# Keys kept on chip, scores read from them in two pieces, loads reordered, and one batch's value sums moved

## The reference

```
k_sum = k.reshape(B,H,nb,32,D).max(axis=3);  v_sum = v.reshape(B,H,nb,32,D).mean(axis=3)
scores_l = scale * q @ k.T      kept where |i-j| < 16, else -1e9
scores_s = scale * q . k_sum + log(32)
a = softmax(concat(scores_l, scores_s));  x = a @ concat(v, v_sum)
x = (silu(x @ w_gate) * (x @ w_val)) @ w_out          # 512 -> 1536 -> 512
h = x @ w_in;  out = g(h) @ w_out2                    # 512 -> 2048 -> 512
```

## Time and profile before

| | us |
|---|---|
| median of 3 runs | 648.65 |
| span of the profiled execution (the page names no other time of it) | 649.1 |
| PE busy | 627.6 |
| DVE, ACT, POOL busy | 356.3, 323.3, 30.4 |
| PE busy from 90 us to the last matmul | without a gap |

### The profile page before, as it was taken

One profiled execution on the slowest core, in us unless ns is written; L12 is line 12 of the kernel. 1 busy time (PEld: TensorE's weight loads), 2 busy tenths in 40 slices (PEclk: granted clock), 3 DMA queues, 4 the chain that ended last, 5 costly groups with the idle time before them and its releaser, 6 DMA issues.

```text
span 649.1 us, 9400 instructions
## 1 busy us (share of the span) xinstructions
PE 627.6 (97%) x3144; PEld 510.9 (79%) x3144; DVE 356.3 (55%) x553; ACT 323.3 (50%) x622; POOL 30.4 (5%) x33
## 2 busy tenths in 40 slices
PE   5779989999999999999999999999999999999997
PEld 2648868888888888888888888888888888888885
DVE  6855455544455555445333447666666666666664
ACT  1844576773468686434333344444444444444442
POOL 3310000100010101000000000000000000000000
PEclk9989979999999999999999999999999999999999
DMA  9997936512922221322332223232253332333221
GB/s 282 261 308 215 223 98 149 160 54 99 253 97 70 75 88 57 97 98 97 97 97 97 65 66 97 97 97 97 97 164 97 97 97 97 125 134 97 97 81 65
DMA packets 49780, 78.51 MB, mean 121 GB/s; under 512 B 16481, under 2 KB 21601, under 8 KB 49505
## 3 DMA queue, kind: packets, MB, share of 16 engines
q1 hardware_dynamic: 49760, 78.27, 39.8%
HBM read 72.48 MB, written 3.15 MB: 117 GB/s over the span
## 4 chain that ended last, share of the span: by engine, by line
PE 88%; SPq 5%; DMA 3%; DVE 1%; ACT 1%; issue 1%; DVEq 0%; ACTq 0%
PE bank L409 49%; PE bank L472 20%; PE bank L454 14%; DMA v_tok<-v_rows_dram 2%; PE bank L344 2%; PE bank L335 2%; SPq L207 2%; DMA win_raw<-w_dram 1%; SPq L203 1%; PE bank L328 1%; PE bank L321 1%; SPq L226 1%; DVE k_sum L681 1%; SPq L233 0%; ACT prob L536 0%
## 5 line engine op out<-in xcount | busy, mean ns | idle before, releaser
L409 PE MATMUL bank<-x_hi,win_hi 128*128 128x512 f32 (+1 forms) x480 | 191.6, 399 | 0.0
L409 PE MATMUL bank<-x_lo,win_hi 128*128 128x512 f32 (+1 forms) x480 | 188.1, 392 | 0.0
L409 PE MATMUL bank<-x_hi,win_lo 128*128 128x512 f32 (+1 forms) x480 | 187.8, 391 | 0.0
L593 ACT ACTIVATE hid_hi<-v_tok 128x512 fp32r<-128x512 f32 x84 | 53.0, 631 | 128.4 <-DVE v_tok L804 75.5
L409 PEld LDWEIGHTS bank<-x_lo,win_hi 128*128 128x128 f32 x480 | 90.7, 189 | 19.4
L409 PEld LDWEIGHTS bank<-x_hi,win_hi 128*128 128x128 f32 x480 | 90.7, 189 | 19.2 <-issue 0.2
L409 PEld LDWEIGHTS bank<-x_hi,win_lo 128*128 128x128 f32 x480 | 90.7, 189 | 18.3 <-issue 0.2
L774 DVE TENSOR_TENSOR hid_lo<-v_tok,hid_hi 128x512 fp32r<-128x512 f32 x84 | 65.5, 780 | 56.1 <-ACT hid_hi L593 56.0
L764 DVE TENSOR_TENSOR win_lo<-win_raw,win_hi 128x512 fp32r<-128x512 f32 (+1 forms) x84 | 76.9, 916 | 19.5 <-ACT win_hi L569 19.5
L472 PE MATMUL bank<-wout_hi,hid_hi 128*128 128x512 f32 x192 | 74.8, 389 | 0.3 <-ACT hid_hi L593 0.3
L472 PE MATMUL bank<-wout_hi,hid_lo 128*128 128x512 f32 x192 | 74.8, 390 | 0.0
(11 more groups left out here) (54 smaller groups left out, 576.4 us busy)
## 6 DMA issues: line engine op xcount, KB each, us to landing
wout_raw<-w_dram SPq DMA_DIRECT2D x84, 256.0 KB, 2.6
win_raw<-w_dram SPq DMA_DIRECT2D x36, 512.0 KB, 4.1
win_raw<-w_dram SPq DMA_DIRECT2D x48, 256.0 KB, 3.0
k_slot<-k_t_dram SPq DMA_DIRECT2D x24, 192.0 KB, 4.7
v_slot<-v_rows_dram SPq DMA_DIRECT2D x24, 192.0 KB, 5.2
v_tok<-v_rows_dram SPq DMA_DIRECT2D x4, 768.0 KB, 8.9
out_dram<-v_slot SPq DMA_DIRECT2D x12, 256.0 KB, 3.0
k_raw<-k_t_dram SPq DMA_DIRECT2D x2, 1056.0 KB, 12.1
```

The costliest lines, as they stand in the source:

```text
L409: last = nc.tensor.matmul(dst[:], a, m, start=k == 0 and i == 0, stop=k == KD - 1 and i == 2)
L593: nc.scalar.activation(hid_hi[:, r], hid[:, r], ACT.Copy).then_inc(hid_hi_ready, 1)
```

## The change

- The keys of both batches get tiles of their own (`k_all`), loaded in three pieces a batch; `k_raw`, `k_slot`, the 24 key DMAs, `place_k_sum` and `load_k_sum` go.
- `scores` makes two products for each pair: 96 columns from `k_all`, 32 from `k_sum`, with the same queries as weights.
- The block maxima are three reductions a batch.
- Load order: keys, first queries, values. The first batch's value sums follow the scores of tiles 1, 2 and 3, and ACT copies them behind the exponentials of tile 3. SP's two `load_v_sum` stay in its list.
- The second batch's values go to `v_late`; their sums come behind the two products of chunk 0.
- Clearing `q_slot` moves from DVE to POOL; the mask has 3 patterns in place of 12; the engines' `Fori` loops are written out.

```diff
-            def load_v_tok(b):
-                if b:
-                    sp.wait_ge(v_sum_done, b)
+            def load_k(b, c):
+                lo, hi = KCH[c]
+                src = k_t[b, :, lo * PAIRS * SUB:hi * PAIRS * SUB]
+                sp.dma_start(k_all[:, b, lo:hi].rearrange("p c a j -> p (c a j)"), src).then_inc(k_loaded[b][c], 16)
...
-            load_v_tok(0)
-            load_k_raw(0, 0)
-            load_k_raw(0, 1)
-            load_qk(0, 0, 2, qk_first_loaded[0])
-            load_qk(0, 2, GRP)
-            load_qk(1, 0, 2, qk_first_loaded[1])
+            load_k(0, 0)
+            load_k(0, 1)
+            load_k(0, 2)
+            load_q(0, 0, 2, q_first_loaded[0])
+            load_v_tok(0)
+            load_q(0, 2, GRP)
             load_v(0)
+            load_q(1, 0, 2, q_first_loaded[1])
+            load_q(1, 2, GRP)
             load_v_sum(0)
-            load_qk(1, 2, GRP)
             load_v(1)
             load_v_sum(1)
-            load_v_tok(1)
...
                 if n == 0:
-                    sp.wait_ge(k_sum_ready, 1)
-                    load_k_raw(1, 0)
-                    load_k_raw(1, 1)
+                    load_v_tok(1)
+                    for c in range(len(KCH)):
+                        load_k(1, c)
...
-            def scores(r, p):
+            def scores(s, p):
+                r, (b, t) = s % SLOTS, divmod(s, TILES)
+                c = t * (QT // SUB)
                 for a in range(PAIRS):
-                    last = nc.tensor.matmul(score_ps[p][:, a], q_slot[:, r, a], k_slot[:, r, :, a],
+                    nc.tensor.matmul(score_ps[p][:, a, 0:WIN], q_slot[:, r, a], k_all[:, b, c:c + WSUBS, a],
+                                     start=True, stop=True)
+                    last = nc.tensor.matmul(score_ps[p][:, a, WIN:], q_slot[:, r, a], k_sum[:, b, :, a],
                                             start=True, stop=True)
...
+                if 1 <= s <= VCH // 2:
+                    value_sums(0, 2 * s - 2)
...
             project(val_ps[0], 0, KD * P, 0).then_inc(in_done, 1)
-            with pe.Fori(0, NBLK - 1) as i:
+            for c in range(0, VCH, 2):
+                value_sums(1, c)
+            for i in range(0, NBLK - 1):
...
-            copy_v_sum(0)
             for s in range(SLOTS):
                 behind(s)
                 act.wait_ge(max_ready, s + 1)
                 exponentials(s)
+                if s == VCH // 2:
+                    copy_v_sum(0)
...
+            def clear_q(c):
+                rows = slice(c * GRP, (c + 1) * GRP)
+                nc.gpsimd.memset(q_slot[0:D, rows, :, QT:], 0.0)
+                nc.gpsimd.memset(q_slot[D:P, rows, :, 0:QT], 0.0).then_inc(q_cleared[c], 1)
```

## The result

| | before | after |
|---|---|---|
| median, us | 649.51 (4 runs, 647.33 to 650.98) | 670.85 (4 runs, 670.28 to 671.0) |
| span of the profiled execution, us | 649.1 | 669.2 |
| PE busy, us (instructions) | 627.6 (3144) | 651.1 (3336) |

The change makes the kernel slower: the ratio after to before is 1.033, with a 95% interval of 1.030 to 1.036. The forecast was 658.7 us with a range of 645 to 664. The direction was right, but the loss is 21.3 us where 10.1 were forecast, and the time lies above the range.

The account below looks back on a forecast made before the run. PE was taken to bound the kernel, busy 627.6 of 649.1 us. Up to chunk 4's scores the terms netted -0.6 us, 12 more tiles added 10.7: +10.1, span 659.2, median 658.7 us, range 645 to 664.

Parts of the forecast that it names:

- The price of a tile: Score products: 16 matmuls a tile, one each 0.11 us, 1.79 us a tile, +0.89.
- The rival of hidden loads: Score products: query loads half as long or not waited for, +0 to +0.25 a tile, 644.1 or 640.5 us; chance 20%.
- (b): Front of the kernel: PE's 2.9 us wait for the values and the slow clock behind it go.
- (c): PE's wait at 85.6 us for late weights: 2.9 us go, and 3.0 us of slow stretch behind it.
- (e): Second batch's value sums behind chunk 0's products: they add 5.2 us; inputs for what follows arrive in time.
- (f): Written-out loops, three masks and fewer DVE clears: no effect on the time.
- Step (d): First eight tiles: PE's work sets the pace, 30.9 us from 9.3, plus two waits; chunk 0 starts at 44.3.
- The wait for the sums: First eight tiles: PE ready for the first values at 28.9, the sums' load landed at 30, 1.1 us.
- The tail: End of the first eight tiles: 7.0 us behind the last scores, PE has 4.2 of work beside it, 2.9 lost.
- The last step of the sum: From profiled span to median: the median lies 0.45 us below the span of 659.2, so 658.7.
- A free front: Front: loads as forecast, but without the two waits and with a quick clock; chunk 0 at 39, 653 to 655 us; 10%.
- The queue behind the sums: SP's queue waits for ACT's copy; 6 us later, first values start at 36 and the result is 664 or more; 12%.

Follow-up runs that it names:

- experiment 1: Kernel before, with each score product of 128 columns made as two, 96 and 32, from the same key slot: 659.45 us, ratio 1.017.
- experiment 4: Kernel after, without the block keys' product for tiles 2 to 23, so eight matmuls of 96 columns remain: 649.89 us, ratio 1.003.
- experiment 7: Kernel after, with 128-column products from key slots filled on chip, first sums' copy one tile earlier, second sums behind values of tiles 5 to 7: 640.99 us.
- Experiment 3: Kernel after, with ACT's copy of the first value sums behind the exponentials of tile 2 in place of tile 3: 664.71 us, ratio 1.025.
- Experiment 5: Kernel after, with the old order at the start: values and first sums ahead of keys and scores: 659.41 us, ratio 1.016.
- experiment 10: Kernel after, with SyncE issuing the second group's values and chunk 0's weights ahead of its wait for the sums: 670.95 us.
- experiment 9: Kernel of experiment 7, with SyncE issuing the second group's values and chunk 0's weights ahead of its wait for the sums: 645.43 us, ratio 0.996.
- 2: Kernel after, with the second batch's value sums moved from behind chunk 0's products to behind the values of tiles 5 to 7: 669.88 us, ratio 1.033.
- 6: Kernel after, with one score product of 128 columns again, from three key slots filled on chip by ACT, DVE and POOL: 646.34 us, ratio 0.998.
- 8: Kernel after, with 128-column products from key slots filled on chip, old order at the start, second sums in the first stage's end: 641.27 us.

## Why the forecast was right in direction and wrong in size

**The price of a tile** was right: 0.90 against 0.89 forecast, taken from the distance of two weight loads in the earlier trace rows. The rival of hidden loads is refuted in three ways: loads that start 0.11 us apart for short and wide products alike, 11.33 in experiment 1, and 10.43 in experiment 4 with a quarter of the columns gone. Two details of the forecast differ: the matmuls themselves are not evenly spaced, and the scores take 1.70 us in the chain for 1.75 to 1.8, since 0.08 of the 0.90 shows in the product behind them. The transposes' short loads in the earlier trace rows did not carry over, as the forecast argued. The section "LDWEIGHTS (loading the stationary operand)" of the Trainium skill's page "TensorE: Matmul & The Clock Gate", by which a load costs its columns over 1.2 ns, agrees: 0.107 by it, 0.111 here. The formula that the forecast took from the section "Back-to-back issue gap" of that page of the Trainium skill is there for an isolated matmul, and the section says that in a stream of loads and matmuls both set the spacing; that agrees with 0.111 us for products of 96 and of 128 columns, and the reading by which the added loads were free does not.

**Steps (b), (c), (e) and (f)** came out as written. The value waits are gone. ACT's idle time for first-layer weights fell from 14.0 to 1.0 us, and PE has no wait near 85 us, nor in experiment 7, whose tiles are as short as before. The second sums cost 5.15 us for 5.2, and nothing behind them was late. Loops, masks and clears cost nothing: PE had no wait for the longer program, and POOL's first two clears took 0.94 and 0.95 us, ahead of 9.9 in any case.

**Step (d) failed, and with it most of the error.** It said "3.0 lost at the slow clock as now", and then two waits. Chunk 0 was to start at 44.3 and started at 54.16, 9.9 us late; at the end of chunk 4's scores it is 102.14 against 92.3, 9.8 late, and 12 tiles at 0.90 follow as forecast. Its terms, with what they measured:

- Start: 9.91 for 9.3, +0.6.
- The first slow stretch: 9.75 us long and full, about half of it lost, 4.9 for the 3.0 charged: +1.9. The 3.0 was taken from a start with twelve dense sums; now short score products stood there.
- The wait for the sums: 1.9 for 1.1. The copy was done at 30.2 for 27, since sums and scores came later with the slow start, and the load took 3.4 us to land: +0.8.
- The slow clock behind that wait: 13.65 us of it with 13.0 of PE work, half lost, 6.5 us. The forecast had no such term.
- The tail: PE idle 2.8 us for 2.9.

These make 9.7 of the 9.9. Experiment 3 takes away the wait (1.9) and the clock's loss behind it (6.5). It started 0.6 earlier, but was slow for 12.0 us at the start (+1.1), and PE was idle for 4.0 us in the tail (+1.2); that makes 6.7, and 6.1 was measured. Experiment 5 shows the rest: start and first slow stretch. It starts 1.8 us ahead of 3 and is slow for 4.1 us in place of 12.0, about 3.9 less lost; that makes 5.7, and its chunk 0 comes 5.6 earlier.

The last step of the sum, "The median lies 0.45 below that span", is the other part. The -0.45 set the median of the kernel before against the span of one of its longer executions; the median after lies 1.65 above its span. Of the 12.1 us between 658.7 and 670.85, 10.0 are in the span and 2.1 in this step; by it alone the time would have stayed in the range.

So the omitted term is the clock, and the reading that should have led to it was at hand. The earlier trace rows showed that a 2.9 us wait cost another 3.0 behind it. The forecast charged such a loss where the trace had one and took it away where a wait went, but placed a new wait of 1.1 us without asking what it would do to the clock, nor whether the products behind it are ones that bring it back.

**The rivals.** "A free front" was wrong in sign. "The queue behind the sums" named the right wait and the right side, but not the mechanism: the copy did come 3 us late, but its condition, values from 36 us on, did not come true (they began at 33.71), and experiment 10 shows that the place of the other loads in the queue is worth nothing in this kernel. The half of it that says "or the load lies behind others" is what experiment 9 made happen. It should have had its own price, wait plus clock, and more than 12%.

**What stays open.** Why the clock comes back so late behind short products is not settled. These rows tell it by what PE executed: with split products in the stretch behind the wait it stayed at 1.2 GHz for some 13.6 us (the kernel after, 2 and 10); with one product for each pair it was back after 3.4 us (4, 6 and 9, though their waits were longer, 3.6 to 4.8). At the start, PE executing split scores first had the fast pace after 9.4 to 12.3 us (after, 2, 3, 4, 10), full scores first after 3.1 to 6.3 (6, 7, 9), sums first after 3.9 to 5.8 (before, 1, 5 and 8). Experiments 4 and 6 remove loads and short streams together, so which of the two holds the clock down is not told apart. Dense products don't always bring it back at once either: the kernel before has one slow stretch of 3.4 us behind its wait for the values, and one of 6.8 us, mostly with dense products, behind its wait for ACT:

```profile
36.80:40.50 3.70, 3.69 (x6) 1.61 (x7) 1.43 (x2) 1.06 (x1) 0.00 (x0) 0.54 1.00 411
84.90:91.70 6.80, 6.13 (x28) 4.97 (x29) 3.65 (x6) 4.27 (x8) 1.04 (x1) 0.50 0.19 62
```

Nor is the least wait that drops it known: 1.9 us did in three kernels, 1.0 to 1.6 us did not in the kernel before (at 20.0), 3, 5, 7 and 8.

## What to carry to other kernels

Splitting the moving operand of a float32 product repeats its weight load. In these rows, once a matmul was shorter than its load, the load was the price: count loads times 0.11 us (128 columns of weights), not columns. When data is to stay on chip but does not lie in one piece, let an idle engine assemble it, and keep the product whole. A wait of TensorE of 1.9 us or more has to be priced here as the wait plus the stretch at half clock behind it; waits up to 1.6 us left the clock up. With split products the start that begins with the dense sums was the better one (experiment 5); with full products the order made no difference once the copy came early (experiments 7 and 8).

## What the hardware showed that was not expected

- TensorE stayed at 1.2 GHz for 13.65 us, and in 13.0 of them the trace has it busy without gaps (granted clock 0.50). The section "What's actually happening" of the Trainium skill's page "TensorE: Matmul & The Clock Gate" says that the gate goes by how busy the array has been; by the profile's busy time alone that does not tell this stretch from the one of experiment 3, which is as busy and ran at 2.4 GHz.
- The clock can fall after a wait is over: in experiments 4, 6, 9 and 10 the granted clock drops 0.4 to 0.9 us after TensorE has started again.
- Two matmuls of 96 columns and two of 32 take 0.447 us together, as four of 128 do, when each has its own load of 128 columns in float32.
- A load of 256 KB that was issued with nothing ahead of it in the queue landed after 3.4 us (`v_sum`, after), and behind values and weights after 7.16 us (experiment 9).
- The granted clock reads 1.00 ahead of the first change on record, though matmuls there run at half pace; at the start of a program the spacing has to be read instead.
